# First loads, key order and the placing of three late tiles in a decay attention, expert and SoLU kernel

## What is computed

```python
# attention with a decaying state; r, k, v are (2, 8, 768, 48)
for t in range(S):
    cur = einsum('bhd,bhe->bhde', u[None] * kt, vt)
    y[:, :, t] = einsum('bhd,bhde->bhe', rt, state + cur)
    state = w[None, :, :, None] * state + einsum('bhd,bhe->bhde', kt, vt)
x = y.transpose(0, 2, 1, 3).reshape(1536, 384)
# router and 8 experts: token i goes to expert_idx[i], the pos-th that does so, kept while pos < capacity (384)
expert_idx = argmax(x @ w_gate, axis=1)
h = maximum(einsum('ecd,edf->ecf', disp, w1), 0);  y = einsum('ecf,efd->ecd', h, w2)
out[i] = gate_w[i] * y[expert_idx[i], pos[i]]
# SoLU block on all tokens
h = x @ w_in;  solu = h * softmax(h);  out = layernorm(solu) * g_ln @ w_out
```

## Time and profile before

| | |
|---|---|
| median of 3 runs | 331.05 us (330.64 to 331.46) |
| profiled execution, its own time | 330.9 us |
| its span, first to last instruction | 329.0 us |
| mean granted TensorE clock | 0.993 |
| PE busy | 312.7 us, 95% of the span |
| DVE, ACT, POOL busy | 63%, 60%, 58% |
| first expert product begins | 83.08 us into the span |

### The profile page before, as it was taken

How to read it: one execution, slowest core, us unless ns; L and a number is a source line. 1 busy time by engine, 2 the same in 40 slices (tenths; PEclk the granted TensorE clock), 3 DMA queues, 4 the chain that set the end, 5 groups by cost and what they waited for, 6 DMA issues and landing times.

```text
span 329.0 us, 6570 instructions
## 1 busy us (share of the span) xinstructions
PE 312.7 (95%) x2380; PEld 281.0 (85%) x2382; DVE 206.0 (63%) x476; ACT 197.4 (60%) x378; POOL 190.0 (58%) x172
## 2 busy tenths in 40 slices
PE   6899998987999999999999999999999999999991
PEld 3688887875899999999999999788999999999991
DVE  4557768798664646464555546899896666655610
ACT  2578776876676676676666767456465444543520
POOL 6976678881878897979798969500131111111221
PEclk9999999999999999999999999999999999999997
DMA  9999999794398948475756585000010000000010
GB/s 130 159 281 265 244 233 281 191 400 152 122 391 293 322 143 290 163 264 185 243 197 230 198 266 209 5 1 2 1 50 0 24 26 24 24 26 25 26 44 27
DMA packets 62898, 50.65 MB, mean 154 GB/s; under 512 B 42512, under 2 KB 58256, under 8 KB 62864
## 3 DMA queue, kind: packets, MB, share of 16 engines
q1 hardware_dynamic: 58896, 45.25, 47.4%
q0 software_dynamic: 1920, 4.73, 3.9%
q10 hardware_dynamic: 2048, 0.22, 0.9%
HBM read 38.37 MB, written 11.82 MB: 153 GB/s over the span
## 4 chain that ended last, share of the span: by engine, by line
PE 75%; issue 7%; POOL 6%; DVE 4%; DMA 3%; ACT 3%; POOLq 0%; DVEq 0%; ACTq 0%; SPq 0%
PE ps L1302 25%; PE ps L1591 15%; PE ps L1574 15%; PE ps L1303 12%; PE ps L1600 3%; POOL own_place L554 2%; ACT scores L749 2%; POOL own_place L558 2%; DMA x_slots<-w_raw,slot 1%; PE ps L1296 1%; DMA wsq<-in_w_dram 1%; POOL place L592 1%; DMA rows_in<-x_slots 1%; DVE own L1001 1%; PE ps L1406 1%
## 5 line engine op out<-in xcount | busy, mean ns | idle before, releaser
L497 POOL TENSOR_TENSOR w_lo<-w_raw,w_hi 128x768 fp32r<-128x768 f32 x33 | 60.4, 1859 | 13.3 <-DVE w_lo L503 12.1
L1302 PE MATMUL ps<-xe,w_hi 128*128 128x448 f32 x192 | 61.8, 378 | 0.3
L1302 PE MATMUL ps<-h,w_hi 128*128 128x448 f32 x192 | 61.6, 377 | 0.0
L1591 PE MATMUL ps<-w_hi,h 128*128 128x384 f32 x192 | 51.5, 340 | 0.0
L1303 PE MATMUL ps<-h,w_lo 128*128 128x224 f32 x192 | 50.8, 264 | 0.0
L1303 PE MATMUL ps<-xe,w_lo 128*128 128x224 f32 x192 | 50.7, 264 | 0.0
L650 POOL TENSOR_TENSOR rstd<-var_b,minus_half 128x1 f32<-128x1 f32 x12 | 6.8, 566 | 72.1 <-DVE var_b L1248 72.1
L1574 PE MATMUL ps<-w_hi,xe 128*128 128x512 f32 x144 | 46.5, 392 | 0.5 <-ACT xe L858 0.5
L936 DVE TENSOR_TENSOR ps<-ps,rk_in 128x448 f32<-128x448 f32 x32 | 20.2, 633 | 36.7 <-ACT rk_in L704 36.7
L1302 PEld LDWEIGHTS ps<-xe,w_hi 128*128 128x128 f32 x192 | 36.0, 187 | 5.0 <-issue 2.3
L1302 PEld LDWEIGHTS ps<-h,w_hi 128*128 128x128 f32 x192 | 36.0, 188 | 2.6
(11 more groups left out here) (162 smaller groups left out, 614.6 us busy)
## 6 DMA issues: line engine op xcount, KB each, us to landing
w_raw<-in_moe_w_dram SPq DMA_DIRECT2D x15, 1536.0 KB, 8.1
x_slots<-zeros SPq DMA_DIRECT2D x6, 768.0 KB, 5.8
rk_in<-in_r_dram SPq DMA_DIRECT2D x12, 192.0 KB, 5.4
rk_in<-in_k_dram SPq DMA_DIRECT2D x12, 192.0 KB, 6.4
v_in<-in_v_dram SPq DMA_DIRECT2D x12, 192.0 KB, 5.7
out_dram<-zeros SPq DMA_DIRECT2D x1, 2304.0 KB, 8.0
w_raw<-in_moe_w_dram SPq DMA_DIRECT2D x3, 512.0 KB, 5.7
rows_in<-x_slots SPq DMA_DIRECT2D x8, 192.0 KB, 8.2
```

Source lines behind the costliest of these rows:

```text
L497: eng.tensor_tensor(w1_lo[:, :, cols], w1_raw[:, i, :, cols], w1_hi[:, :, cols].bitcast(F32), ALU.subtract).then_inc(g.w1_lo, 1)
L1302: pe.matmul(ps[:, bank, 0:2 * n], w_hi, x[:, c, 0:2 * n], start=first, stop=False, skip_group_check=True)
L1591: last = pe.matmul(ps[:, OB + i, 0:DM], ht[:, f, i * P:(i + 1) * P], wt[:, f, :], start=(f == 0 and z == 0), stop=(f == KF - 1 and z == 2))
```

## The change

- SP issues r of tile 0, then one half of w, then k; ACT issues only the other half. ACT fills `pick_pair` (four ACTIVATEs) ahead of issuing u and w_gate. Two of the three pad memsets go from POOL to DVE.
- The odd diagonals of tile 0 are written by DVE; the counters of `diag_ready` follow (`diagonals`).
- In POOL's tiles 5 and 8 the wait for `slot_ready` stands ahead of `last_keys`. In tile 6 ACT takes k before x.
- Three tiles are late, 9 to 11. `columns_of` lies in `scores`. Their slots, needed only by the scatters, are formed together at the end; PE waits for the rank alone. SP's load of rows waits for 9 scatters, where it waited for 10.
- Of the 9 `keep_warm` products in the tail one stays. The first `lo_w2` goes from ahead of L930 to behind the second sum of expert 0.

```diff
-        LATE = [NT - 2, NT - 1]
+        LATE = [NT - 3, NT - 2, NT - 1]
+        columns_of = scores[:, 0].rearrange("p a h t -> p (a h t)")[:, 0:3 * N1].rearrange("p (t n) -> p t n", t=3)
@@ SP load_tile, POOL start, ACT start
                     sp.dma_start(rk_in[:, i, j, :, 0:D], src[b, c]).then_inc(loaded[i], 16)
+                    if t == 0 and j == 0:
+                        sp.wait_ge(wcol_ready, 1)
+                        load_w(sp, 1)
-            pool.memset(rk_in[:]...[:, :, D:DP], 0.0).then_inc(pads_ready, 1)
-            pool.memset(v_in[:]...[:, :, D:DP], 0.0).then_inc(pads_ready, 1)
+            load_w(act, 0)
+            act.wait_ge(ident_ready, 2)
+            act.wait_ge(pick_step, 1)
+            for g in range(2): ...   # the four ACTIVATEs of pick_pair, as they stood behind the issue of g
             act.dma_start(u_all[:]...)
@@ POOL tiles
                 if t < NT - 1:
+                    for n, g in enumerate(GROUPS):
+                        if t == g[-1] + 3:
+                            pool.wait_ge(slot_ready, n + 1)
                     last_keys(t + 1)
...
-                        if t == g[-1] + 3:
-                            pool.wait_ge(slot_ready, n + 1)
                     own_parts(t + 1)
@@ ACT tiles
-                put_diagonal(t, 1)
+                    put_diagonal(t, 1)        # now only for t > 0
+                if t == NC:
+                    take_k(t + 1)
                 if t > 0:
                     take_x(t - 1)
@@ DVE
+            def put_first_diagonal():
+                dve.wait_ge(own_ready, 1)
+                for p in range(HP):
+                    last = dve.tensor_scalar(scores[:, 0, 1, p, :], ident[:], own[:, 2 * p + 1:2 * p + 2], None, ALU.mult)
+                last.then_inc(first_odd_ready, 1)
+            def rank_late(j):      # waits picked and counts; tensor_tensor_reduce -> rank, then_inc(late_rank, 1)
+            def late_columns(j):   # slot_a; wait; tensor_scalar(columns_of[:, j], column_key, slot_a, is_equal)
+            def late_slots():      # slot_b and slot of the three tiles, two instructions; then_inc(slot_ready, 3)
-            place_tokens(len(GROUPS) - 2)
+            late_columns(0)
+            rank_late(1)
             add_picked(len(GROUPS) - 2)
             take_logits(NT - 1)
             pick_experts(len(GROUPS) - 1)
-            place_tokens(len(GROUPS) - 1)
+            late_columns(1)
+            rank_late(2)
+            late_columns(2)
+            late_slots()
             add_picked(len(GROUPS) - 1)
             lo_w1(dve, 0, 0, usual, parts=[1, 2])
-            lo_w2(dve, 0, 0, usual, 0)
             dve_first_xe_lo(dve)
...
+                if e == 0:
+                    dve_h_sum(dve, e, usual, [0])
+                    dve_h_lo(dve, e, usual, [0])
+                    dve_h_sum(dve, e, usual, [1])
+                    lo_w2(dve, 0, 0, usual, 0)
@@ PE tail
             count_before(len(GROUPS) - 2)
-            keep_warm(2, RT)
             split_x(NT - 1)
             place_late(0)
             count_before(len(GROUPS) - 1)
-            keep_warm(3, RT)
             place_late(1)
+            place_late(2)
             place_first_rows()
...
-            keep_warm(4, OB)
+            keep_warm(1, OB)
```

More of the change, by code:

```diff
@@ L353, in updates, with diagonals @@
             return t + 1 - (t + 1) // NC
+        def diagonals(t):
+            return max(2 * t - 1, 0)
         def y_half(h):
@@ L715, in _ @@
             act.wait_ge(wcol_ready, 1)
-            w_pairs = w.rearrange("(p g) d -> g d p", g=2)
+            load_w(act, 0)
+            act.wait_ge(ident_ready, 2)
+            act.wait_ge(pick_step, 1)
             for g in range(2):
-                act.dma_start(wsq[DP * g:DP * g + D, 0, :, 0], w_pairs[g],
-                              allow_slow_non_contiguous=True).then_inc(w_dma, 16)
+                for odd in range(2):
+                    rows = y_half(2 * odd + g).start
+                    act.activation(pick_pair[:, odd::2, D * g:D * g + D],
+                                   ident[:, rows:rows + D].unsqueeze(1).to_broadcast([P, HP // 2, D]), ACT.Copy)\
+                        .then_inc(pick_ready, 1)
             act.dma_start(u_all[:].rearrange("p h d -> p (h d)"),
@@ L728, in _ @@
                           allow_slow_non_contiguous=True).then_inc(g_in, 16)
[L731 to L738, removed]
             act.wait_ge(wlast_turned, 1)
@@ L790, in _ @@
                 if t < NT - 1:
-                    take_k(t + 1)
+                    if t != NC:
+                        take_k(t + 1)
                     put_diagonal(t + 1, 0)
@@ L999, in add_own @@
                 if t > 0:
-                    dve.wait_ge(diag_ready, 2 * t)
+                    dve.wait_ge(diag_ready, diagonals(t))
                 dve.tensor_reduce(own[:], ruk[:], AX_X, ALU.add).then_inc(own_ready, 1)
+            def put_first_diagonal():
[3 more added lines that the diff above has]
+                last.then_inc(first_odd_ready, 1)
             def mask_scores(t):
@@ L1006, in mask_scores @@
                         lo_w1(dve, 0, 0, usual, parts=[0])
-                    dve.wait_ge(diag_ready, 2 * t + a + 1)
+                    if t == 0 and a == 1:
+                        dve.wait_ge(first_odd_ready, 1)
+                    else:
+                        dve.wait_ge(diag_ready, diagonals(t) + a + 1)
                     dve.wait_ge(scores_done, 2 * t + a + 1)
@@ L1061, in place_tokens @@
                 dve.wait_ge(counts_done, n + 1)
[L1062 to L1069, removed]
+                dve.tensor_tensor(rank_e[:, g], counts(size), picked[:, g], ALU.mult).then_inc(rank_step, 1)
+                dve.wait_ge(rank_step, 4 * n + 1)
+                dve.tensor_reduce(rank[:, g], rank_e[:, g], AX_X, ALU.add).then_inc(rank_step, 1)
                 dve.wait_ge(rank_step, 4 * n + 2)
@@ L1074, in place_tokens @@
                 dve.wait_ge(rank_step, 4 * n + 4)
[L1075 to L1078, removed]
                 dve.scalar_tensor_tensor(out=slot[:, g], in0=slot_a[:, g], scalar=float(E * CAP), in1=slot_b[:, g],
                                          op0=ALU.add, op1=ALU.add).then_inc(slot_ready, 1)
+            def rank_late(j):
+                t, n = LATE[j], group_of(LATE[j])
+                dve.wait_ge(picked_ready, n + 1)
+                dve.wait_ge(counts_done, n + 1)
+                dve.tensor_tensor_reduce(out=rank_e[:, t, :], in0=ps[:, UB, CNT:CNT + E], in1=picked[:, t, :], scale=1.0,
+                                         scalar=0.0, op0=ALU.mult, op1=ALU.add, accum_out=rank[:, t:t + 1]).then_inc(late_rank, 1)
+            def late_columns(j):
+                t = LATE[j]
+                dve.wait_ge(late_rank, j + 1)
+                dve.scalar_tensor_tensor(out=slot_a[:, t:t + 1], in0=top[:, t:t + 1], scalar=-float(CAP), in1=rank[:, t:t + 1],
+                                         op0=ALU.mult, op1=ALU.add).then_inc(late_slot_a, 1)
+                dve.wait_ge(late_slot_a, j + 1)
+                if j == 0:
+                    dve.wait_ge(key_ready, 2)
+                    dve.wait_ge(y_done, NT - 1)
+                dve.tensor_scalar(columns_of[:, j], column_key, slot_a[:, t:t + 1], None, ALU.is_equal).then_inc(columns_ready, 1)
+            def late_slots():
+                g = slice(LATE[0], LATE[-1] + 1)
+                dve.tensor_scalar(slot_b[:, g], rank[:, g], float(CAP), BIG, ALU.is_ge, ALU.mult).then_inc(late_slot_b, 1)
+                dve.wait_ge(late_slot_b, 1)
+                dve.scalar_tensor_tensor(out=slot[:, g], in0=slot_a[:, g], scalar=float(E * CAP), in1=slot_b[:, g],
+                                         op0=ALU.add, op1=ALU.add).then_inc(slot_ready, len(LATE))
             def add_picked(n):
@@ L1110, in _ @@
                     if t == g[-1] + 2:
-                        place_tokens(n)
+                        if g[-1] in LATE:
+                            rank_late(LATE.index(g[-1]))
+                        else:
+                            place_tokens(n)
                         add_picked(n)
-            place_tokens(len(GROUPS) - 2)
+            late_columns(0)
+            rank_late(1)
             add_picked(len(GROUPS) - 2)
```

28 lines of the change are left out of this document (19 added, 9 removed).

## The result

The changed kernel takes 329.34 us in the median of 5 runs (328.78 to 329.82), the kernel before beside it 330.76 (330.02 to 331.46): ratio 0.9952, 95% interval 0.9934 to 0.9970. By the ratio that is 1.6 us less (1.0 to 2.2); the two medians differ by 1.4. The profiled execution has a span of 327.6 us, 1.4 less than before.

What follows compares the result with a forecast made beforehand. PE is busy nearly throughout the expert stretch, so only the first expert product's start counts. Start 0, k before x 0, keys behind slots -0.45, tail -1.2, handover 0 sum to -1.65: 329.4 us, range 328.4 to 330.9.

Steps and rivals of the forecast that it cites:

- little arrives: Rival, chance 0.18: ACT's diagonals hide the slot gain, the tail gives only 0.7, handover costs 0.3; 330.6 us.
- the start comes through: Rival, chance 0.07: tile 6's loads land earlier too and u is no obstacle; 1.4 us more gain, 328.0 us.
- Start, term 0: Tile 0: u lands late, `own_parts(0)` at 8.8; output 0.1 us late, hidden by tile 6; ends 0 and +0.7.
- The rival that POOL holds DVE: Tile 0, chance 0.08: DVE's first diagonals each end only with a POOL product, 1.5 us late; 330.3 us.
- None of this arrives: Tile 0's shift never reaches the end: tile 6 still waits for k at 37.36, idle time in tile 7 absorbs lateness.
- k before x, term 0: Tile 6 loads: PE's hole before tile 7's products moves to the count behind them; 0, ends 0 and -0.3.
- Keys behind slots, -0.45: Tile 8: short slot instructions remove PE's 0.64 us idle, `own(9)` 0.45 us earlier, handed through to tile 11; ends 0 and -0.65.
- Tail, -1.2: From tile 11's last split to the first expert product: split 0.85 earlier, rows' product 0.95, then 0.25; ends -0.7 and -1.5.
- Limited by PE, no more by memory: Tail: rows land at 79.5, PE is ready at 80.05, so `place_first_rows` starts 0.95 us earlier.
- -0.25 for the fill products and `lo_w2`: Between `place_first_rows` and the first expert product: 0.54 us of fill products and late rests goes, of which 0.25 was taken.
- Handover, 0: Expert 0: POOL's w2 rests start about 2 us later, later 2.2 late, without PE waiting; ends 0 and +0.5.
- Clock: Rival, chance 0.07: TensorE falls to its lower clock between 10.0 and 14.5, tile 1's products double; 334 us.

Runs made afterwards that it cites:

- the start alone: Kernel before with only the changed loads, memsets and tile 0's odd diagonals on DVE; ratio 1.0002 (0.9981 to 1.0024) to the kernel before.
- run 7: Changed kernel with DVE's four first diagonals reading the identity from PSUM and loads of tiles 5 to 8 ahead of the zeros; ratio 0.9969 to the kernel before.
- run 6: Changed kernel with the loads of tiles 5 to 8 issued ahead of the zeros; ratio 0.9968 to the kernel before.
- run 4: Changed kernel with all eight first diagonals back on ACT; ratio 0.9939 to the kernel before.
- run 11: Changed kernel with POOL's wait for the choice of experts also ahead of the key product (tiles 4, 7, 10); ratio 0.9954 to the kernel before.
- run 8: Changed kernel with the first `lo_w2` back ahead of the first rests of x on DVE; ratio 0.9972 to the kernel before.
- run 12: Changed kernel with POOL's wait for the choice also ahead of the keys and all eight first diagonals on ACT; ratio 0.9952 to the kernel before.
- run 5: Changed kernel with DVE's four first diagonals reading a copy of the identity in PSUM, not SBUF; ratio 0.9974 to the kernel before.

## Why the prediction was right, point by point

329.4 was forecast, 329.34 measured; the sum of -1.65 stands against -1.4 in the span and -1.6 (1.0 to 2.2) by the ratio. The agreement of the whole is closer than that of its parts, and in so far luck: at the fourth expert block the two profiles differ by 0.24 us up to t6 (forecast 0), 0.34 from t6 to t11 (0.45) and 0.98 behind it (1.2). The 330.6 of "little arrives", 0.45 us less than before, lies outside the interval, and the start alone (1.0002) doesn't bring the 1.4 us of "the start comes through".

**Start, term 0: right in size, partly wrong in reason.** u was the last to come, as said, but at 7.6 us, not 8.8: ACT's queue issued it at 3.21, when the first ACTIVATE had only begun, and I had put it behind all four. In nine further profiles with this start, `own_parts(0)` lies between 7.72 and 8.25, without it between 8.16 and 8.51 (four). Of the 0.52 us the diagonals take back 0.34; 0.18 is left at t0. The rival that POOL holds DVE was true in its mechanism: 2.50 us against 1.13. I had argued against it from 0.34 us for 224 columns, which I took for the pace of any other, and that was misread: from PSUM the same kind of instruction took 0.34 for 128 columns, and from SBUF, where nothing held it, 0.27. Its price was too high. Of the 1.5 us that I gave it 0.6 was u's lateness and 0.9 the hold; against ACT's eight the stretch is 0.3 to 0.4 longer. The first was held only by the product already running and the fourth slipped into a gap, 1.4 us together, and the masks that follow ran as a pair. The Trainium skill (GPSIMD Engine Reference, "Key points") names a DVE instruction with two SBUF inputs or in a 2-port mode as the one that contends. The runs agree with it: held were these, faster from SBUF (0.27 us) than from PSUM (0.34), and small instructions with two inputs from SBUF such as `slot_a`, but not the sum `own`.

**"None of this arrives"** was too strong. Fourteen profiles say when it does. In the ten in which POOL's key product of tile 6 started up to 22.8 us behind t0 (run 7 aside), t6 followed t0 by 30.83 to 30.90 us, PE's own pace (30.85 in run 6, where k was there 5 us ahead of its use). Behind some 22.7, t6 is late by the excess:

| profile | keys of tile 6 - t0 | t6 - t0 |
|---|---|---|
| run 4, run 11, changed | 22.53, 22.58, 22.68 | 30.85, 30.90, 30.84 |
| before | 22.80 | 30.90 |
| run 8 | 23.15 | 31.26 |
| run 12 | 23.85 | 31.98 |
| run 5 | 24.29 | 32.41 |
| run 7 | 22.74 | 31.05 |

(Runs 5 and 7 lose 0.2 us already in tile 1, 5.45 us for 5.27.) The kernel before stood on that edge in its first profile, as I read in the earlier trace rows; in its second the distance is 22.07. In the twelve profiles with the old order of the zeros k of tile 6 landed between 36.42 and 37.77, with no regard to the start's part (36.42 and 37.77 are runs 4 and 12, whose t0 is 14.07 and 14.04). Whether an earlier start counts is decided by the loads of each execution. I had not seen that the new wait also stands ahead of tile 6's keys: the slots of group 0 let them go at 22.5 to 22.7, on the edge, and cost nothing in these profiles.

**k before x, term 0:** held. The hole moved, to the split (0.31) and not only to the count.

**Keys behind slots, -0.45:** the place held to the row (`slot_a` 0.16, keys at 52.82, no 0.64). Tile 9's output is 0.5 us nearer t6 than in before's two profiles on average (16.77 against 17.28). In six of the nine profiles with the new order it lies 16.59 to 16.81 behind t6, in the five with the old order 16.85 to 17.83; the other three (runs 5, 7 and 12: 17.38, 18.72, 17.74) had late loads or zeros. Past that, profiles can't tell: t11 - t6 is 27.40 against 27.74 and 27.41. In the changed kernel PE waits 0.98 us for ACT's yt ahead of tile 10's split, where it was 0.65 and 0.78. The times speak for a gain only weakly: 0.7 us alone (0.0 to 1.3). POOL's `last_keys(11)` holds DVE in group 2's choice just as `last_keys(9)` held `slot_a`, which I had missed, but it did so in the kernel before too (1.33 and 1.56 us for `below`, which otherwise takes 0.18), so it isn't what took a gain back.

**Tail, -1.2: right as a sum, its limit named wrongly.** From t11 to the first expert product it is 8.75 us instead of 9.88, -1.13; to the fourth block 10.02 instead of 11.00, -0.98. The split gained 0.85 against t11, as forecast. The rows' product gained 0.66 and not 0.95, and the way from there to the first expert product 0.47 (0.32 to the fourth block) and not 0.25. The 1.13 us for a placing behind another stands in no row; two took 2.54. "Limited by PE, no more by memory" fell. I had let the scatter of tile 8 land in the 4.13 us of tile 9's. From the last needed scatter's issue to SP's load it took 3.3 to 4.1 us in the four profiles with the old tail, and 3.4 to 6.2 in those with the new one (5.07 in the changed kernel, whose load was issued at 77.08). Of the ten profiles with the new tail four waited for rows (0.27, 1.24, 0.61, 0.38 us) and a fifth is the changed kernel: its bracket shows no wait, but its second load of rows, issued at 77.46, took 2.2 us to land at about 79.6, and the product came 0.24 later than in the five that reached 6.88 to 6.89 behind t11. In those five PE was the limit, as forecast. The last scatter that the load needs was issued 1.9 us earlier than before (72.01 and 73.94), but 0.9 us of that went in the longer way to the load. The -0.25 for the fill products and `lo_w2` was too small: 0.47, of which the pace of ACT's high parts, 0.45 us for each of the first blocks, takes 0.15 back. Run 8 puts the part of `lo_w2` at 0.1 or nothing. The fill products were not tried alone.

**Handover, 0:** held. POOL was 2.4 us later against PE (forecast 2.2), PE had no idle time. POOL's wait in expert 1, 2.56 before, took up 1.4 of it; 1.0 stayed and cost nothing there:

```profile
98.88 3.65 POOL L512 TENSOR_TENSOR w_lo<-w_raw,w_hi 128x768 fp32r<-128x768 f32 x2 [1.17 <-DVE w_lo L518]
```

**Clock:** the stretch 10.0 to 14.5 had PE busy for 2.43 us, less than the 3.01 of the earlier trace rows, and kept 1.00, so this rival did not come about.

**Left over:** the fourth block was 1.56 us earlier, the end 1.4. The difference arises where the experts hand over to SoLU: PE is idle 0.73 us there (before 210.29), where it was 0.51.

The gain at the fourth block by parts, in these two profiles: 0.18 us at t0, 0.06 more to t6, 0.34 from t6 to t11, 0.98 behind it. The 0.34 is the size of the difference between two profiles of one kernel, and only the 0.98 stands well above that.

What stays open: what spreads the landings, k's in tile 6 by 1.35 us and the scatters' by 2.9. No run took one transfer alone away from beside them. The eight variants of the changed kernel lie between 0.9939 and 0.9974, with intervals that overlap.

## What to carry to other kernels

Take work off one engine only after looking at what the helping engine's operands share with a third: four multiplications that looked free took 2.50 us instead of 1.13 because POOL was at work on SBUF. When a compute stage gets earlier, find for each load and scatter whether its issue gets earlier with it. Where a load lands just when it is needed (here k of tile 6, needed some 22.7 us behind tile 0's output), the gain arrives in some executions and not in others. A part's gain is read best over a short distance in which two profiles of one kernel agree (here 0.04 us over the tail), and from medians where they don't.

## What the runs showed of the hardware

- A DVE instruction with a tensor from SBUF and a scalar for each token was held by POOL's tensor products: four 128x128 took 2.50 us, 1.13 with the tensor in PSUM. One that nothing held took 0.27 from SBUF, 0.34 from PSUM.
- Small DVE instructions with two inputs from SBUF, 0.16 to 0.18 us by themselves, took up to 1.32 (`slot_a`) and 1.83 (`lscore`, run 4) when they met POOL's products (1.0 us, and 0.6 behind it). DVE's sum of 384 columns from SBUF took 0.53 to 0.56 with such a product beside it or not.
- ACT's queue issued u's load at 3.21, with the first of four ACTIVATEs begun at 3.20 and the last ending at 4.00: an issue behind ACTIVATEs in program order did not wait for their ends.
- With w's two halves in two queues, the last landed at about 4.2 (1.30 + 2.9; DVE's wait for it ended at 4.25), not at 4.93.
- The same chain, scatter to load issue, took between 3.3 and 6.2 us in profiles of nearly equal kernels.
